# Decayed attention ahead of a mixture of experts: chunks of 64 tokens on four 64x64 array tiles, and a loop in TensorE's program

## What is computed

```python
scores = scale * np.matmul(q, k.transpose(0, 1, 3, 2))
Dmat = np.where(rel >= 0, gamma[:, None, None] ** rel[None, :, :], 0.0)
x = np.matmul(scores * Dmat[None, :, :, :], v)      # then rows of 512 per token
logits = x @ phi                                    # 4608 tokens, 32 slots
d = exp(logits - max over tokens) / its sum         # dispatch weights
slot_input = d.T @ x                                # then eight experts: relu(. @ w1) @ w2
c = exp(logits - max over slots) / its sum          # combine weights
x = c @ slot_out
out = ((x @ w1) * (x @ w2)) @ w3 @ w_out
```

## Time and profile before

| | us |
|---|---|
| median of three runs | 391.99 |
| the profiled execution | 393.09 |
| its span, first to last instruction | 391.3 |
| `x_t` of tile 8 ends | 39.65 |
| `x_t` of tile 36, the last, ends | 159.26 |
| fold and experts end, about | 250 |

### The profile page before, as it was taken

The page is one execution under the profiler, slowest core; times in us unless marked ns, Lnnn a source line. Parts: engine busy times, 40 slices in busy tenths (PEclk is TensorE's granted clock), DMA queues, the critical chain, the costliest instruction groups (busy, mean ns, idle before and its releaser), DMA issues. The chain is left out here.

```text
span 391.3 us, 10219 instructions
## 1 busy us (share of the span) xinstructions
PE 368.7 (94%) x4215; PEld 275.1 (70%) x4215; DVE 160.4 (41%) x278; ACT 128.4 (33%) x249; POOL 165.3 (42%) x159
## 2 busy tenths in 40 slices
PE   3889999998989899899999999899999999999996
PEld 2878686876777758564656555468878888888885
DVE  1554475455545546161013000699843323233320
ACT  1022312321322122522334220522733454434442
POOL 1562242223213321544536450397955554545530
PEclk9999999999999989999999999999999999999999
DMA  7997999899889985869999991048226655556222
GB/s 249 394 372 257 382 392 360 283 401 398 317 330 356 354 299 211 299 262 365 382 391 418 422 415 74 2 96 233 92 83 228 225 199 183 192 174 237 113 107 107
DMA packets 37884, 104.25 MB, mean 266 GB/s; under 512 B 3988, under 2 KB 6484, under 8 KB 34004
## 3 DMA queue, kind: packets, MB, share of 16 engines
q1 hardware_dynamic: 37844, 103.66, 71.9%
HBM read 93.32 MB, written 10.32 MB: 265 GB/s over the span
## 5 line engine op out<-in xcount | busy, mean ns | idle before, releaser
L654 POOL TENSOR_TENSOR feat<-c_sb 128x512 f32<-128x512 f32 x45 | 56.6, 1269 | 46.4 <-PE psum L1037 44.3
L1246 DVE TENSOR_TENSOR weights_t<-psum,const_sb 128x512 f32<-128x512 f32 x72 | 46.3, 684 | 32.0 <-PE psum L689 32.0
L595 POOL TENSOR_TENSOR pkg_sb<-pkg_sb,const_sb 128x512 f32<-128x512 f32 x27 | 28.2, 1043 | 70.9 <-DMA pkg_sb<-in_tiles 70.9
L1037 PE MATMUL psum<-m_hi,feat_hi 128*128 128x512 f32 x144 | 56.1, 390 | 0.3 <-DVE m_lo L1468 0.3
L1037 PE MATMUL psum<-m_lo,feat_hi 128*128 128x512 f32 x144 | 56.0, 389 | 0.0
L1037 PE MATMUL psum<-m_hi,feat_lo 128*128 128x512 f32 x144 | 56.0, 389 | 0.0
L432 DVE TENSOR_TENSOR feat_lo<-feat,feat_hi 128x512 fp32r<-128x512 f32 x34 | 27.3, 802 | 62.1 <-ACT feat_hi L1182 61.0
L1182 ACT CAST feat_hi<-feat 128x512 fp32r<-128x512 f32 x45 | 27.9, 622 | 39.0 <-POOL feat L654 39.0
L628 POOL TENSOR_TENSOR w_lo<-fold_raw,w_hi 128x512 fp32r<-128x512 f32 x16 | 20.7, 1296 | 46.0 <-ACT wo_hi L1114 46.0
L1056 ACT COPY state_sb<-psum 128x256 f32<-128x256 f32 x32 | 11.9, 373 | 76.8 <-PE psum L738 76.8
L689 PE MATMUL psum<-pkg_sb 64*64 64x128 f32 (+1 forms) x864 | 27.4, 262 | 8.0 <-DMA pkg_sb<-in_tiles 6.6
(11 more groups left out here) (138 smaller groups left out, 570.8 us busy)
## 6 DMA issues: line engine op xcount, KB each, us to landing
pkg_sb<-in_tiles SPq DMA_DIRECT2D x59, 256.0 KB, 5.9
pkg_sb<-in_tiles SPq DMA_DIRECT2D x23, 512.0 KB, 6.5
c_sb<-c_rows SPq DMA_DIRECT2D x45, 256.0 KB
unit_a<-in_units SPq DMA_DIRECT2D x11, 1024.0 KB, 11.1
unit_x<-in_units SPq DMA_DIRECT2D x9, 1024.0 KB, 8.0
out<-out_sb SPq DMA_DIRECT2D x36, 256.0 KB, 2.1
fold_raw<-in_fold SPq DMA_DIRECT2D x12, 512.0 KB, 6.6
unit_a<-in_units SPq DMA_DIRECT2D x12, 512.0 KB, 7.3
```

The costliest lines, as they stand in the source:

```text
L595: nc.gpsimd.tensor_tensor(v_nat(g, t).rearrange("p (h d) -> p h d", h=HEADS), v_nat(g, t).rearrange("p (h d) -> p h d", h=HEADS), decay.un ...
L654: nc.gpsimd.tensor_tensor(feat[:, k, :], c_sb[:, s, x, :], c_sb[:, s, y, :], ALU.mult).then_inc(feat_ready, 1)
L1037: last = mm(psum[:, OUT + b, :], x, y, start=(at == 0 and m == 0), stop=(at == 4 and m == 2))
L1246: tt(weights_t[:, (2 * t + odd) % 4, :].rearrange("p (k b n) -> p k b n", k=2, b=2), psum[:, odd, :].rearrange("p (k b n) -> p k b n", k=2 ...
```

## The change

The chunk becomes 64 tokens. All attention matmuls are then 64x64 weights with 64 columns, on four 64x64 tiles of the array:

- `scores`: 16 matmuls, only the two diagonal blocks of a tile; one mask instruction of 128x512 in place of two.
- `update` (new, in place of `state`): 16 matmuls give each half's product of k and v alone, in banks 4 and 5. DVE adds it to the carried state (`next_state`, two instructions of 128x256 per tile, into a ring of eight states); ACT's `copy_state` goes.
- `through_states`: 16 matmuls of 64 columns. `through_scores`: 16, in two phases of 8; between the phases stand `turn_x` and `logits` of the tile before.
- `logits` runs per tile, `x_t` as weights and phi as 32 columns, so that logits come in token rows; ACT copies them (`copy_logits`). `turn_softmax` goes: DVE turns 32x32 blocks (`nc.vector.transpose`) in `max_logits` and `turn_exp`. The maximum over a slot is folded over four row blocks by eight small copies.
- `dispatch`: four column tiles in place of three, 8 matmuls of 512 columns and 4 of 128. Its sums are copied by ACT, no longer by DVE.
- `x_t` holds two tiles in place of nine, `x_nat` is a ring of 12, and `pkg_sb` holds all four tile places.
- PE's program for the first four tiles is written out; tiles 5 to 36 are a loop of eight turns of four tiles (`Fori`), with `If` around `dispatch` and around the last look-ahead. The other engines stay written out.
- In the tail, `fold(4)` and `fold(2)` with two small matmuls between them become `fold(5)`, and ACT makes the split of part group 1 (`split_hi(1)`) behind the last exponential, no longer ahead of it.

```diff
-            def state(g, t):
...
-                for h in range(HEADS):
-                    a, r = h // 2, HD * (h % 2)
-                    last = mm(bank[r:r + HD, a, :], k_nat(g, t)[:, HD * h:HD * (h + 1)],
-                              v_nat(g, t)[:, HD * h:HD * (h + 1)],
...
+            def update(n, r):
...
+                        cols = slice(HD * (2 * a + odd), HD * (2 * a + odd + 1))
+                        for half in range(2):
+                            rows = slice(HD * half, HD * (half + 1))
+                            last = mm(psum[HD * odd:HD * (odd + 1), UPDATE + half, HD * a:HD * (a + 1)],
+                                      k_nat(r)[rows, cols], v_nat(r)[rows, cols], start=True, stop=True)
...
+            def logits(n, r):
...
                 for a in range(PAIRS):
+                    last = mm(psum[:, RAW, 0:SLOTS], x_t[:, r % 2, a, :], phi_sb[:, a, :],
+                              start=(a == 0), stop=(a == PAIRS - 1))
...
+                through_states(n, r)
+                through_scores(n, r, 0)
+                if not is_first(n):
...
+                    before = (r + SLOTS_IN - 1) % SLOTS_IN
+                    turn_x(n - 1, before)
+                    logits(n - 1, before)
+                through_scores(n, r, 1)
+
+            scores(0, 0, 16)
+            update(0, 0)
+            for r in range(SLOTS_IN):
+                step(0, r)
+            with pe.Fori(1, NTILES // SLOTS_IN) as i:
+                for r in range(SLOTS_IN):
+                    step(i, r)
...
+            def next_state(c):
...
+                    dve.wait_ge(states_ready, c + 1)
+                    tt(to, new, state_sb[:, c % STATES_IN, :, :].rearrange("p a n -> p (a n)"),
+                       ALU.add).then_inc(states_ready, 1)
...
+            mask_scores(0)
+            next_state(0)
+            next_state(1)
+            for n in range(NTILES):
+                g, t = divmod(n, TILES)
+                if n < NTILES - 1:
+                    mask_scores(n + 1)
+                    next_state(2 * n + 2)
+                    next_state(2 * n + 3)
+                if g > 0 and t == 1:
+                    turn_exp(g - 1)
+                scale_x(n)
+                if g > 0:
+                    if t == 0:
+                        max_logits(g - 1)
+                    if t == 2:
                         shift_combine(g - 1)
-                    if not is_first(g) and t == 3:
-                        copy_sums(g - 1)
+                    if t == 4:
                         finish_combine(g - 1)
```

More of the change, by code:

```diff
@@ L43 @@
 SLOTS, EXPERTS, FF = 32, 8, 1024
-SUBS = 3
-SUB = TILES * P // SUBS
+SUBS = 4
 NFEAT = (SLOTS // 2 + 1) * SLOTS
@@ L685, in scores @@
                         for half in range(2):
-                            later = half == (0 if a >= 2 else 1)
-                            lo = HD if later and not first else 0
-                            last = mm(psum[HD * half:HD * (half + 1), odd, P * a + lo:P * (a + 1)],
-                                      k_t(g, t)[rows, a, HD * half:HD * (half + 1)], q_t(g, t)[rows, a, lo:P],
+                            cols = slice(HD * half, HD * (half + 1))
+                            last = mm(psum[cols, odd, HD * a:HD * (a + 1)], k_t(r)[rows, a, cols], q_t(r)[rows, a, cols],
                                       start=True, stop=True)
@@ L743, in turn_x @@
-            def turn_x(g, t):
-                if is_first(g) and t == 0:
+                        cols = slice(HD * (2 * a + odd), HD * (2 * a + odd + 1))
[3 more added lines that the diff above has]
+                                      k_nat(r)[rows, cols], v_nat(r)[rows, cols], start=True, stop=True)
+                            if a == PAIRS - 1:
+                                last.then_inc(update_ready[half], 1)
@@ new lines, in out_of, with through_states @@
+            def out_of(a, odd, half):
+                r, c = HD * (a % 2), P * (a // 2) + HD * half
+                return psum[r:r + HD, OUT_T + odd, c:c + HD]
+            def through_states(n, r):
+                if not is_first(n):
+                    pe.wait_ge(x_t_ready, n)
+                pe.wait_ge(states_ready, n * 2 + 2)
+                begin(n)
+                for half in range(2):
+                    for a in range(PAIRS):
+                        for odd in range(2):
+                            rows = slice(HD * odd, HD * (odd + 1))
+                            mm(out_of(a, odd, half), state_sb[rows, 2 * r + half, a, :],
+                               q_t(r)[rows, a, HD * half:HD * (half + 1)],
+                               start=(half == 0 and a < 2), stop=True, skip_group_check=True)
@@ new lines, in through_scores @@
+            def through_scores(n, r, phase):
+                if phase == 0:
+                    pe.wait_ge(masked, n + 1)
+                else:
+                    pe.wait_ge(phase_done, n * QUARTERS + QUARTERS)
+                begin(n)
+                for a in range(PAIRS):
+                    for half in range(2):
+                        odd = half if phase == 0 else 1 - half
+                        rows, h = slice(HD * half, HD * (half + 1)), 2 * a + odd
+                        last = mm(out_of(a, odd, half), v_nat(r)[rows, HD * h:HD * (h + 1)],
+                                  weights_t[rows, r % 2, odd, HD * a:HD * (a + 1)],
+                                  start=False, stop=True, skip_group_check=True)
+                        if a >= PAIRS - 2:
+                            last.then_inc(phase_done if phase == 0 else out_ready, 1)
@@ L791, in dispatch @@
-                last.then_inc(sums_ready, 1)
-            def group(g):
-                scores(g, 0)
-                if not is_first(g):
-                    turn_x(g - 1, TILES - 1)
-                    logits(g - 1)
-                for t in range(TILES):
-                    if t < TILES - 1:
-                        scores(g, t + 1)
-                    if t > 0:
-                        through_state(g, t)
-                    for turned in TURNS[t][:-1]:
-                        turn_x(g, turned)
-                    through_scores(g, t)
-                    if t < STATES:
-                        state(g, t)
-                    if not is_first(g) and t == 1:
-                        turn_softmax(g - 1)
-                    if not is_first(g) and t == 3:
-                        dispatch(g - 1)
-                    for turned in TURNS[t][-1:]:
-                        turn_x(g, turned)
```

560 lines of the change are left out of this document (255 added, 305 removed).

## The result

The changed kernel takes 430.61 us, the median of four runs (429.95 to 433.04), and the kernel before took 390.56 on the same chip: a ratio of 1.103 with a 95% interval of 1.098 to 1.108. It is slower by 40 us, where a small gain was forecast, and outside the range given. The profiled execution of it took 429.95, with a span of 428.2.

The account below looks back on a forecast made before the run. PE and DMA both almost full in the last 28 tiles, plus waits for 256-instruction blocks; first eight tiles +9.9, other 28 −11.8, tail −0.5, total −2.4 us, so 390 us, range 378 to 415.

Parts of the forecast that it names:

- The loop is kept: PE's loop: its 5.2 blocks of 256 instructions stay held, so no instruction packets come from tile 8 to tile 36.
- The three blocks seen held: Loop in the earlier trace: at least three instruction blocks held across branches back; five or six were not shown.
- The passes: PE's attention matmuls: 64-column passes on four array tiles start 14.5 ns apart, 128 per tile, 1.86 us.
- rival 2's first half: PE passes miss 14.5 ns; at 22.5 a tile takes 4.3 us, time 418; rivals 2 and 4 together 0.20.
- Sum ... 3.34 us: PE per tile: passes 1.86, turn 0.44, logits 0.48, shapes 0.4, `x_t` 0.1, registers and branches 0.06.
- The logits: PE per tile: 8 passes loading 128 weight columns for 32 streamed, 0.48 us, between 0.2 and 0.9.
- The sequencer: PE's registers and branches: about 0.2 us per branch, mostly hidden while queued matmuls run; 0.06 us per tile.
- rival 2's second half: PE sequencer's ISA, ALU and branch steps show between blocks of work; rivals 2 and 4 together 0.20.
- the 8 that I had given: Last 28 tiles: DVE stalls of 3 × 2 = 6 us and 2 us for late data.
- 4.3 us each ... 49.5 us: First eight tiles: 10 new blocks, about two covered to 14.5 us, 8.2 at 4.3 us; end 49.5 (44 to 60).
- Rival 4: First ten blocks' fetches cost 6.5 us each behind a full queue: +18, time 408; rivals 2 and 4 together 0.20.
- Sum −0.5 us: Tail: turns and small matmuls save 1.2 us, dispatch 0.6, fifth fold part waits about 1.5; range −3 to +2.

Follow-up runs that it names:

- e_more_incs: Changed kernel with two more semaphore increments at each call of `begin` in PE's loop, fourteen more per tile; 464.02 us.
- a_fold3: Changed kernel with fold(3) in place of fold(2) ahead of the experts, so 12 fold parts stand there as before the change; 420.09 us.
- c_unrolled: Changed kernel with all 36 tiles of PE's program written out, no loop; 474.21 us.
- j_half_data: Written-out kernel (all 36 tiles on PE) with only a sixteenth of k and q turned loaded from the fifth tile on; 450.31 us.
- b_early_loop: Changed kernel with PE's loop begun at tile 2 instead of tile 5, one tile written out, nine turns; 424.49 us.

## Why the prediction was wrong

**The loop is kept: right.** Ten packets until tile 8 ends, none from there until tile 36. The three blocks seen held in the earlier trace rows were a fair sign.

**The passes: right.** 15 ns against 14.5, and so rival 2's first half, slower passes at 22.5 ns, falls, and with it the 25 ns per matmul of the Trainium skill (TensorE: Matmul & The Clock Gate, Back-to-back issue gap): on four 64x64 tiles the passes start closer than that.

**"Sum ... 3.34 us": failed, 3.80 at the least and 4.00 in the mean.** Two terms. The logits: 0.91, not 0.48. Each pass loads 128 columns of weights for 32 columns streamed, and costs 111 ns, the same as a turn's; the upper bound of 0.9 was the truth, since the row nearest in the size of its *weights* was the turn, and I had weighed it by what it streams. The sequencer, in the tile of 4.08 us shown above: 128 passes at 15 ns are 1.9 us, and the five attention pieces take 2.67 (0.67 + 0.49 + 0.37 + 0.50 + 0.64), so 0.77 lies between pieces, where I had 0.56 (0.4 for two shapes, 0.1 for `x_t` and 0.06 for registers and branches); in the tile with the branch back 0.3 more. `e_more_incs` shows that such steps are exposed, which is rival 2's second half. I had priced them as hidden behind queued matmuls. My reading, not tested, is that they hide only while a piece runs longer than the steps of the next: 16 passes of 64 columns, at 15 ns each, last 0.24 us.

Over 28 tiles 0.66 × 28 = 18.5 us. All else in them, DVE's group stalls, late data and what dispatch took above its 6.3, came to 2.7 instead of the 8 that I had given (121.0 − 28 × 4.00 − 6.3), so the 28 tiles came out 13.2 above the forecast.

**"4.3 us each ... 49.5 us": failed, 64.08.** The number of blocks was right. The first wait for a block ended at 18.3, not at 14.5: +3.8. The next eight blocks took 41.1 us, to 59.44, or 5.1 each in place of 4.3: +6.7, with the wait of 4.64 in it. The last fifth of a block took 4.6 in place of 0.9, at the lower clock: +3.8. That is 14.3 of the 14.6. I had argued that an emptier data queue makes a fetch shorter. Where it was nearly empty (DMA share under 0.2, four blocks) the next packet did come 1.0 to 1.3 us after PE entered a block, but from the packet on PE needs 2.2 to 3.0 more, and at 52.8 to 56.6 the queue was full again. The low clock (0.50 in 20 to 26 and 33 to 50) looks like the culprit in the rows, and from 37.4 to 54.8 no block was late: PE itself took 5 us for each. But most of the time that the clock costs is time in which PE would have waited for the next block: kernels with two and with four such tiles reach tile 8 together. Rival 4 named the mechanism, at 6.5 us a block, and gave 408 for it.

**"Sum −0.5 us" in the tail: failed, +11.2.** The step looked at the first five fold parts. Their waits came in other sizes: the first, still on POOL, was 2.43 us in place of 0.29, and the fifth 0.43 in place of 1.5. That is small beside what the step left out: it did not count what the new calls of `fold` add up to. The phase is worth 10.5 in `a_fold3`. This term alone was to be had from the diff: 12 parts before, 11 after, and a buffer that turns over every 4.

With the tail alone wrong the time would have been 402, inside the range; all three together put it outside. Two of the three signs of being wrong that the prediction named came: tile 8 behind 60 us, and a tile above 3.7. The loop did what it is for, and yet the 28 tiles take 121.0 us where they took 119.6: the waits for instructions are gone, but the halved causal work is paid back by logits in eight short passes and by more pieces for the sequencer. No variant that does all the work beat the kernel before; the best is 24 us above it.

## What to carry to other kernels

Count PE's instructions ahead of a loop as well as in it: here each 256 new ones took 5.0 to 5.5 us, those that a branch jumps over counted too, a body of 5 blocks was kept and one of 10 was not. Where matmuls come in pieces of a few hundred nanoseconds, every increment between them added its own length or more, and a short pass cost what its weight load suggests (111 ns for 128 columns loaded, whether 32 or 128 were streamed). And when the number of calls of a double-buffered producer is edited, add the calls up modulo the group: a remainder of one cost 10 us in a stage that the change never touched.

## What was not expected of the hardware

- A fetch of a 16 KB block has two parts: the packet starts 0.8 to 4.0 us after PE enters the block ahead, and at a wait PE goes on 2.2 to 3.2 us after the packet's start (`c_unrolled`), 0.9 to 1.7 of them for the packet. The second part is as long when the DMA engines have less to do (2.0 to 2.9 in `j_half_data`).
- PE's granted clock fell to its 1.2 GHz level four times in the record: at 19.5 us, 1.2 behind a wait of 2.07; at 33.2, behind one of 0.70; at 57.1, within the wait of 4.64; and at 186.8, within the one of 2.43. The kernel before saw one such stretch, at 135.7 to 139.1.
- A 1.00 of the page at the start of a trace need not be the granted clock. In `b_early_loop` the first record of the clock is of 28.15 us, and the page gives what lies ahead of it as 1.00, while the eight logits passes there take the 1.75 us of the lower level. In the changed kernel the records begin at 16.09. The passes' own length tells more:

```profile
20.00:25.00 5.00, 5.00 (x102) 4.82 (x102) 1.03 (x3) 0.77 (x2) 2.05 (x2) 1.00 0.12 43
```
```profile
22.29 1.75 PE L751 MATMUL psum<-phi_sb,x_t 128*128 128x32 f32 x8
```

Left open: what the 1.2 to 1.6 us between the end of a packet and PE's next instruction are, what an increment costs beyond its own record, and where between 5.2 and 10.4 blocks the loop stops being kept.
